# Softmax bias and scale from a two-column DVE operation on negated scores, in place of two POOL operations on the row maximum

## The reference

```python
q_bucket = np.sum(q_bits * powers, axis=-1)      # from the signs of q @ proj, 6 bits
k_bucket = np.sum(k_bits * powers, axis=-1)
mask = q_bucket[:, :, :, None] == k_bucket[:, :, None, :]
scores = scale * np.matmul(q, k.transpose(0, 1, 3, 2))
scores = np.where(mask, scores, -1000000000.0)
scores = scores - np.max(scores, axis=-1, keepdims=True)
attn = np.exp(scores)
attn = attn / (np.sum(attn, axis=-1, keepdims=True) + 1e-09)
return np.matmul(attn, v)
```

## Time and profile before

| | |
|---|---|
| median of 3 runs | 871.3 us (870.92 to 872.27) |
| the profiled execution, its own time | 870.19 us |
| span of the profiled execution | 868.5 us |
| attention, from the first score to the last weighted product | 18.6 to about 292 us |
| PE busy, whole span | 785.9 us, 90% |
| DVE busy | 399.4 us, 46% |
| ACT busy | 338.7 us, 39% |
| POOL busy | 380.7 us, 44% |

### The profile page before, as it was taken

One profiled execution on the slowest core, in us unless ns is written; L12 is line 12 of the kernel. 1 busy time (PEld: TensorE's weight loads), 2 busy tenths in 40 slices (PEclk: granted clock), 3 DMA queues, 4 the chain that ended last, 5 costly groups with the idle time before them and its releaser, 6 DMA issues.

```text
span 868.5 us, 13829 instructions
## 1 busy us (share of the span) xinstructions
PE 785.9 (90%) x4070; PEld 662.3 (76%) x4071; DVE 399.4 (46%) x693; ACT 338.7 (39%) x671; POOL 380.7 (44%) x462
## 2 busy tenths in 40 slices
PE   3899999999999509999999999948999999999998
PEld 2788898898889407888887777836888888888886
DVE  2887888788788601222122212204344443434333
ACT  1777777777777302222222222222232222322222
POOL 1533443343344179499999999239300000000000
PEclk9999999999999858999999999978999999999999
DMA  6575474354444055465666666324000100000001
GB/s 158 136 208 142 117 214 122 92 137 118 120 107 108 5 190 185 131 195 195 201 196 195 191 199 191 115 64 146 13 25 13 48 0 0 0 19 31 1 1 48
DMA packets 71212, 95.05 MB, mean 109 GB/s; under 512 B 32144, under 2 KB 34192, under 8 KB 71184
## 3 DMA queue, kind: packets, MB, share of 16 engines
q1 hardware_dynamic: 63792, 78.44, 30.8%
q10 hardware_dynamic: 5472, 9.96, 3.4%
q0 software_dynamic: 1920, 6.29, 2.1%
HBM read 59.54 MB, written 16.25 MB: 87 GB/s over the span
## 4 chain that ended last, share of the span: by engine, by line
PE 67%; issue 12%; POOL 7%; DMA 6%; DVE 4%; SPq 1%; ACT 1%; POOLq 1%; DVEq 0%
PE ps_s L626 9%; PE ps_s L628 9%; PE ps_s L627 9%; PE ps_t L579 6%; PE ps_t L724 5%; PE ps_t L726 5%; PE ps_t L725 5%; PE ps_o L591 4%; PE ps_o L592 4%; POOL w_lo L485 3%; PE ps_s L562 3%; PE ps_s L563 3%; POOL w_hi L481 2%; PE ps_p L545 2%; DMA late_stage<-in_moe_w_dram 2%
## 5 line engine op out<-in xcount | busy, mean ns | idle before, releaser
L791 ACT ACTIVATE probs<-ps_s,stats 128x768 f32<-128x768 f32 x96 | 95.3, 992 | 26.5 <-POOL stats L435 26.0
L938 DVE TENSOR_REDUCE stats<-ps_s 128x1 f32<-128x768 f32 x96 | 91.5, 953 | 25.5 <-PE ps_s L563 25.2
L951 DVE TENSOR_TENSOR pt_lo<-ps_t,pt_hi 128x384 fp32r<-128x384 f32 x192 | 97.0, 547 | 9.9 <-ACT pt_hi L784 9.6
L433 POOL TENSOR_SCALAR stats<-stats 128x1 f32<-128x1 f32 x96 | 21.1, 220 | 152.1 <-DVE stats L938 151.9
L579 PE MATMUL ps_t<-ident,probs 128*128 128x128 f32 x576 | 82.6, 277 | 5.1 <-DVE pt_lo L951 5.0
L784 ACT ACTIVATE pt_hi<-ps_t 128x384 fp32r<-128x384 f32 x192 | 83.4, 490 | 7.9 <-PE ps_t L579 7.5
L485 POOL TENSOR_TENSOR w_lo<-stage,w_hi 128x1024 fp32r<-128x1024 f32 x36 | 86.5, 2403 | 0.0
L485 POOL TENSOR_TENSOR w_lo<-late_stage,w_hi 128x1024 fp32r<-128x1024 f32 x36 | 86.1, 2408 | 0.0
L562 PE MATMUL ps_s<-key_hi_hi,query_lo_hi 128*128 128x384 f32 x192 | 69.9, 364 | 10.3 <-DMA finish<-in_moe_w_gate_dram 8.2
L724 PE MATMUL ps_t<-yT_hi,w_hi 128*128 (+1 forms) x192 | 77.0, 401 | 2.2 <-DVE yT_lo L1090 1.4
L579 PEld LDWEIGHTS ps_t<-ident,probs 128*128 128x128 f32 x576 | 65.8, 141 | 16.4 <-DVE pt_lo L951 14.1
(11 more groups left out here) (146 smaller groups left out, 1606.5 us busy)
## 6 DMA issues: line engine op xcount, KB each, us to landing
stage<-in_moe_w_dram SPq DMA_DIRECT2D x72, 256.0 KB, 2.9
late_stage<-in_moe_w_dram SPq DMA_DIRECT2D x56, 256.0 KB, 3.0
key_hi_hi<-query_hi_mask SPq DMA_DIRECT2D x32, 192.0 KB, 3.8
x_slots<-x_rows SPq DMA_DIRECT2D x19, 256.0 KB, 3.8
xg<-x_slots ACTq DMA_DIRECT2D x19, 256.0 KB, 3.2
y_slots<-y_sb ACTq DMA_DIRECT2D x19, 256.0 KB, 2.7
raw_qk<-in_q_dram SPq DMA_DIRECT2D x16, 192.0 KB, 3.2
raw_qk<-in_k_dram SPq DMA_DIRECT2D x16, 192.0 KB, 3.9
```

The source lines that it names most:

```text
L951: v_.tensor_tensor(pt_lo[gb][where], ps_t[:, half, 0:HW].rearrange("p (t c) -> p t c", c=P), pt_hi[gb][where].bitcast(F32), ALU.subtract). ...
```

## The change

The query rows of `qk_hi` and `qk_lo` are multiplied by -1/8 when they leave PE's bank (`side`, one column of 128 values: -1/8 for the query partitions, 1 for the key partitions). The scores then arrive in `ps_s` as minus the scaled score, with a positive mask of 2^100 (two factors of 2^50). DVE takes the row minimum, and a second DVE operation on two columns multiplies the pair (minimum, -1) in `stats` by (minimum < 2^99), which is 1 or 0; the two products are what the exponential reads as bias and scale. The signs of the projection are turned to match. POOL's two operations and their semaphores go. `stats` grows by one column per slot. Four memsets of `amp` are replaced by two of `side` and one of `stats`.

```diff
-        stats, c = place("stats", [P, 3, 4], F32, c)
+        stats, c = place("stats", [P, 4, 4], F32, c)
...
-        amp, c = place("amp", [P, 1], F32, c)
+        side, c = place("side", [P, 1], F32, c)
...
# POOL
-                        c = slice(s % 4, s % 4 + 1)
-                        wait_apart(max_found, n + 1)
-
-                        g.tensor_scalar(stats[:, 1, c], stats[:, 0, c], -BIG / 2, SCALE, ALU.is_gt, ALU.mult).then_inc(scale_ready, 1)
-                        wait_apart(scale_ready, n + 1)
-                        g.tensor_scalar(stats[:, 2, c], stats[:, 0, c], stats[:, 1, c], -1.0, ALU.mult, ALU.mult).then_inc(bias_ready, 1)
...
+            pool.wait_ge(made, 5)
             pairs(pool, body)
...
# ACT
-                a(qk_hi[j][:, half * HW:(half + 1) * HW], bank[:, 0:HW], ACT.Copy).then_inc(qk_hi_moved, 1)
+                a(qk_hi[j][:, half * HW:(half + 1) * HW], bank[:, 0:HW], ACT.Copy, scale=side[:]).then_inc(qk_hi_moved, 1)
...
-                          bias=stats[:, 2, c], scale=stats[:, 1, c], accum_out=sums[:, j, u:u + 1]).then_inc(exp_done, 1)
+                          bias=stats[:, c, 2:3], scale=stats[:, c, 3:4], accum_out=sums[:, j, u:u + 1]).then_inc(exp_done, 1)
...
+            act.wait_ge(proj_split, 1)
             move_qk(0, 0, 0, ps_p)
...
# DVE
-                v_.tensor_tensor(qk_lo[j][:, cols], bank[:, 0:HW], qk_hi[j][:, cols].bitcast(F32), ALU.subtract).then_inc(prep_moved, 1)
+                v_.scalar_tensor_tensor(qk_lo[j][:, cols], bank[:, 0:HW], side[:], qk_hi[j][:, cols].bitcast(F32), ALU.mult, ALU.subtract).then_inc(prep_moved, 1)
...
-                v_.tensor_scalar(bits[:, half * HW:(half + 1) * HW], bank[:, 0:HW], thr[:], amp[:], ALU.is_gt, ALU.mult).then_inc(prep_moved, 1)
+                v_.tensor_scalar(bits[:, half * HW:(half + 1) * HW], bank[:, 0:HW], thr[:], HALF_BIG, ALU.is_gt, ALU.mult).then_inc(prep_moved, 1)
...
-                        v_.tensor_reduce(stats[:, 0, c], ps_s[:, 2 * (s % 2):2 * (s % 2) + 2, 0:HW], AX.XY, ALU.max).then_inc(max_found, 1)
+                        v_.tensor_reduce(stats[:, c, 0:1], ps_s[:, 2 * (s % 2):2 * (s % 2) + 2, 0:HW], AX.XY, ALU.min).then_inc(least_found, 1)
+                        dve.wait_ge(least_found, n + 1)
+                        v_.scalar_tensor_tensor(stats[:, c, 2:4], stats[:, c, 0:1].to_broadcast([P, 2]), BIG / 2, stats[:, c, 0:2],
+                                                ALU.is_lt, ALU.mult).then_inc(bias_ready, 1)
...
-            for q, (test, size) in enumerate(((ABOVE, 1.0), (NOT_ABOVE, 1.0), (NOT_ABOVE, -BIG), (ABOVE, -BIG))):
+            for q, test in enumerate((ABOVE, NOT_ABOVE, NOT_ABOVE, ABOVE)):
                 v_.memset(thr[q * 32:q * 32 + 32, :], test)
-                v_.memset(amp[q * 32:q * 32 + 32, :], size)
+            v_.memset(side[0:D, :], -SCALE)
+            v_.memset(side[D:P, :], 1.0)
+            v_.memset(stats[:, :, 1:2], -1.0)
...
-                for q, sign in enumerate((1.0, -1.0, -1.0, 1.0)):
+                for q, sign in enumerate((-1.0 / SCALE, 1.0 / SCALE, -1.0, 1.0)):
```

More of the change, by code:

```diff
@@ L48, in attention_moe_mlp @@
     BIG = 2.0 ** 100
+    HALF_BIG = 2.0 ** 50
     PROJ_SCALE = 2.0 ** 24
@@ L214, in attention_moe_mlp @@
         split_v_hi, v_split = sem("split_v_hi"), sem("v_split")
-        scale_ready, scored, max_found, bias_ready, exp_done = sem("scale_ready"), sem("scored"), sem("max_found"), sem("bias_ready"), sem("exp_done")
+        scored, least_found, bias_ready, exp_done = sem("scored"), sem("least_found"), sem("bias_ready"), sem("exp_done")
         guarded, inverted = sem("guarded"), sem("inverted")
@@ L786, in body @@
                     if live(i, s, 0, UNITS):
-                        c = slice(s % 4, s % 4 + 1)
+                        c = s % 4
                         act.wait_ge(bias_ready, n + 1)
```

## The result

The changed kernel takes 881.46 us (median of 4 runs, 879.9 to 881.9) against 871.5 us before, a ratio on record of 1.0122 with a 95% interval of 1.0109 to 1.0134: about 10.6 us slower. The plain quotient of the two medians is 1.0114, or 10.0 us; in the experiments, too, the ratio on record and the quotient of the medians differ by up to 0.1%. I had forecast slower with 87%, and 877.7 us. The median lies within the range given, 873.9 to 882.0; the kernel before times the ratio, 882.1, lies just beyond it. In the profiled execution the span grew from 868.5 to 878.2 us.

A forecast was written before the change was run, and what follows sets the result against it. PE, busy 90% of the span, was taken as the bound, paying DVE's latency from reduction to pt_lo. 2.9 + 3.2 + 0.25 = 6.4 us on the median 871.3 gave 877.7 us, range 873.9 to 882.0.

The forecast's parts named there:

- The sign: Whole kernel: slower by more than the 1.7 us a measurement can tell, given 87%.
- u = 4: Reduction, new operation, reciprocal, pt_lo, PE: nothing absorbs the addition, 14 heads x 0.21 = 2.9 us.
- u = 1 into 2: Later qk_lo and pt_lo delay PE's transposes past 0.04 us of slack: 14 heads x 0.23 = 3.2 us.
- The price of the operation: On DVE behind each reduction: 0.21 us more per unit, 0.12 for the later start and 0.09 for the operation.
- The lower end: New DVE operation costs only 0.09 us if its wait for the reduction is free; the time is then 874.4 us.
- POOL's 192 operations go: POOL in the attention: removing its operations was counted at nothing, since it was off the chain.
- ACT does not cover it: In u = 1, ACT moves qk_hi at 106.21, so qk_lo was waiting for DVE alone.
- The start and the last heads: Start: qk_lo on the chain, +0.25 us; last head: counted 0, between -0.9 and +0.4 us.
- the earlier exponential: Exponential some 0.7 us sooner after the reduction; almost nothing waits for it, but 0.4 us to gain twice in the last head.
- The faster rival: Earlier exponential lets x_rows out earlier and ends PE's 7.6 us of waits for it: 866.8 us, 7%.

The follow-up runs named there:

- e3: Kernel before, plus a two-column DVE operation behind each row maximum that waits for it, result unused: ratio 1.0088 to before.
- e4: Kernel before, plus the same kind of two-column DVE operation, but on constants and without the wait for the reduction: ratio 1.0036 to before.
- e1: Changed kernel with POOL made to wait for each unit's bias before going on: ratio 1.0092 to the kernel before.
- e2: Changed kernel with minimum and constant in spare PSUM columns, so the two-column operation has one SBUF input; empty-bucket test left out: ratio 1.0103 to before.
- e6: Changed kernel with a one-column Copy on ACT ahead of its first real one, so the table load comes early: ratio 1.0107 to before.
- e5: Changed kernel with the two-column operation moved behind qk_lo, the bits or the reciprocal, ahead of pt_lo: ratio 1.0104 to before.
- e9: Kernel before with the scaling alone: ACT's move to qk_hi and DVE's qk_lo multiply by a column of ones: ratio 1.0019 to before.
- e10: Like e7, but the reduction negates its maximum and queries and keys are multiplied by a constant, without scaling columns; POOL paced: ratio 1.0012 to before.
- e7: Changed kernel with POOL paced, table load early, two-column operation later (in u = 4 behind pt_lo, with the reciprocal): ratio 1.0028 to before.

## Why the prediction was right or wrong

- **The sign, and that PE pays for DVE's latency: right.** Slower was forecast with 87%. The two places, u = 4 and u = 1 into 2, both showed in the chain, and e3, which holds nothing but the added operation, gave 1.0088.
- **The price of the operation: right.** 0.21 us was taken in u = 4, 0.20 to 0.21 measured (0.97 to 1.18 for `pt_lo`), 0.13 of it the wait. Both halves came from neighbouring rows. The lower end, where the wait costs nothing, as the Trainium skill's rule would have it, was refuted by e3 against e4.
- **u = 1 into 2: mis-sized, by a wrong path.** The term was 0.23 us a head, by `pt_lo` and the second half of `ps_t`. It measured 0.30: in the heads without a long operation the reduction of u = 4 starts 11.59 us after `x_rows`, before 11.29. The path is `qk_lo` to the projection, which stands earlier in PE's program and had even less slack, 107.31 to 107.38 us. I looked at the consumer that the list of waits named, and not at every consumer of what DVE produces there. With both places, 14 x 0.50 is 7.0 us instead of 6.1. Such a head is 0.55 us longer than the mean before (17.53 against 16.98); the last 0.05 come behind the reduction of u = 5, and I did not trace them.
- **"POOL's 192 operations go: it was off the chain and only does its splits of v and of weights sooner", priced at nothing: this is the step that failed.** It cost about 3 us over the heads 1 to 12, by e1 and by e2 (2.4 if e6 is put in the place of the change), of a loss that was 10.0 to 10.6 us where 6.4 was forecast. The POOL operations that went had also paced those that stayed, and the new DVE operation is the only one in the slots whose inputs both lie in SBUF. Neither was in the sum, nor among the rivals, and the range had no room for it.
- **"ACT does not cover it": right in the change, not in general.** ACT's 0.09 us were priced at nothing, and in the change they are hidden behind the two-column operation. As soon as that moved (e5) or was absent (e9), ACT was the one that came last.
- **The start and the last heads: not told.** 0.25 us was forecast for the start and 0.38 measured until the rows of head 0, but over all thirteen kernels this point lies anywhere from 50.5 to 53.0 us, one execution each, so the agreement says little. The late table load I had not seen in the order of ACT's instructions; it costs nothing that e6 could tell. For the last heads 0 was counted, between -0.9 and +0.4, and 0.4 measured: the gain by the earlier exponential did not show.
- **The faster rival is refuted.** The exponential does come earlier: ACT's waits for its bias fell from 21.4 to 6.1 us in the stretch of the earlier trace rows. But PE's wait for `x_rows` grew from 7.6 to 8.8 us, and no wait of PE that was read became shorter.

## What to carry to other kernels

Where a DVE step is on PE's path between its wait for scores and its next matmul, an added small operation costs its own 0.07 us, and 0.13 us more if it must wait for the reduction ahead of it, each time. Before work moves from POOL to DVE, ask what the moved instructions had been holding back, and whether the new DVE operation has both inputs in SBUF while POOL works: then it lasts until POOL's operation is over, and pacing POOL or keeping one input in PSUM removes it. And a step on the chain is only worth what separates it from the next one in line: the 0.09 us of the reciprocal bought nothing, while 0.2 us added next to it cost in full.

## What the runs showed of the hardware that was not expected

- A DVE operation on two columns, 0.16 us, took up to 1.05 us in the change beside a POOL operation when both its inputs were in SBUF, and 0.16 us beside the same one when one was in PSUM. A TENSOR_SCALAR of 64x6 with one input, in SBUF, took 0.49 instead of some 0.16 us beside POOL's split of v (e6), while a reciprocal of 128x6 kept its 0.18 us beside POOL (e2).
- A scale from a column of SBUF, where there was none, costs ACT 0.09 us on 128x384 (0.49 to 0.58) and DVE's `qk_lo` 0.06 to 0.07 (0.55 to 0.62). A constant in the instruction costs neither anything that shows (0.49 and 0.56 in e10).
- PE's clock at the end of the attention differs between executions. In the last product of e10 the mean granted clock from 291 to 296 us was 0.68, while the kernel before had it full (2.4 GHz) until 296; the rows are those of the windows, of e10 and then of the kernel before (length, busy PE, PEld, DVE, ACT, POOL, then the clock):

```profile
291.00:296.00 5.00, 3.53 (x12) 3.02 (x12) 0.95 (x3) 0.76 (x2) 0.00 (x0) 0.68 0.00 0
```

```profile
291.00:296.00 5.00, 3.71 (x24) 3.28 (x23) 0.52 (x2) 0.49 (x1) 0.00 (x0) 1.00 0.00 0
```

Read in steps of 1 us, the clock in e10 was full until 292, 0.88 from there to 293, 0.50 (1.2 GHz) to 296 and 0.92 to 297. PE, busy all the time, began 5 matmuls from 293 to 294; the kernel before began 7 from 291 to 292. From the rows of head 14 to those of head 15 this made 9.99 instead of 8.84 us in e10, and 10.2 to 10.4 in e1, e7 and e9. PE had stood nearly idle just before, waiting for `pt_lo` of the last units (busy 0.09 of the microsecond from 291 in e10), but so it had in the kernel before (0.20 of that from 290), whose clock stayed full. What decides it stays open; it is 1.2 to 1.5 us in the profiled executions of these four, which is why their heads were compared and not their spans.
